# A banded attention and two mixture-of-experts layers on one core: lane weights in halves, other stretches of products, lists inside the third tile, another order of the first units

## The reference

```python
k_sum = k.reshape(B, H, nb, 32, D).max(axis=3); v_sum = v.reshape(B, H, nb, 32, D).mean(axis=3)
# scores: q k^T inside a band of |i-j| < 16, and q k_sum^T + log 32 for the 24 blocks; softmax over both
x = a @ concat(v, v_sum)                      # -> 3072 tokens x 512
# layer 1, closed experts of 384 places: all 3072*8 logits x @ w_gate in falling order,
#   each token goes to the first expert that still has a place
out[mask_e] = relu(x[mask_e] @ w1[e]) @ w2[e]                    # w1 512x1024, w2 1024x512
# layer 2: tokens with x @ w_skip > 0 only, e = argmax(x @ w_gate), gate = softmax at e
out[mask_e] = x[mask_e] + gate * (relu(x[mask_e] @ w1[e]) @ w2[e])
```

## Time and profile before

| | |
|---|---|
| runs without profile | median 840.15 us of 3 (838.03 to 840.93) |
| profiled execution | 839.7 us, its span 837.9 us |
| PE busy | 800.1 us, 95% of the span |
| DVE, ACT, POOL busy | 460.3, 228.3, 214.9 us |
| chain that ended last | PE 76%, DVE 12%, DMA 5%, issue 2%, POOL 2% |
| largest PE groups | L1482 184.0 us, L1496 179.8 us, L1612 102.6 us, L1630 98.8 us |

### The profile page before, as it was taken

The page is one execution under the profiler, slowest core; times in us unless marked ns, Lnnn a source line. Parts: engine busy times, 40 slices in busy tenths (PEclk is TensorE's granted clock), DMA queues, the critical chain, the costliest instruction groups (busy, mean ns, idle before and its releaser), DMA issues.

```text
span 837.9 us, 15121 instructions
## 1 busy us (share of the span) xinstructions
PE 800.1 (95%) x4996; PEld 512.7 (61%) x4996; DVE 460.3 (55%) x2113; ACT 228.3 (27%) x681; POOL 214.9 (26%) x313
## 2 busy tenths in 40 slices
PE   7999998998999999999999999999999999999996
PEld 6778786885445455454554545555576686777762
DVE  7889896777777766667766677516058000000000
ACT  6878786501112021121212212121111111110101
POOL 6888973001030210202102030120300321211110
PEclk9999999999999999999999999999999999999999
DMA  9986650716070622507135070437978999898983
GB/s 252 283 246 206 218 157 6 258 62 222 0 289 26 218 96 71 218 25 264 51 119 194 1 289 25 165 150 278 345 306 330 398 360 348 309 341 305 331 321 115
DMA packets 64505, 171.66 MB, mean 205 GB/s; under 512 B 5584, under 2 KB 5584, under 8 KB 64448
## 3 DMA queue, kind: packets, MB, share of 16 engines
q1 hardware_dynamic: 54512, 143.70, 49.5%
q0 software_dynamic: 6480, 20.91, 6.4%
q10 hardware_dynamic: 3456, 6.29, 2.0%
HBM read 148.41 MB, written 22.81 MB: 204 GB/s over the span
## 4 chain that ended last, share of the span: by engine, by line
PE 76%; DVE 12%; DMA 5%; issue 2%; POOL 2%; SPq 1%; ACT 1%; DVEq 0%; POOLq 0%; ACTq 0%
PE bank L1496 19%; PE bank L1482 16%; PE bank L1630 12%; PE bank L1612 11%; DVE junk L1035 6%; PE bank L1345 3%; PE bank L1372 3%; PE bank L1354 2%; DMA kc<-in_kT 2%; PE bank L1562 1%; DMA weights<-in_moe_w 1%; PE bank L1688 1%; DVE reached L1050 1%; DVE cand L1052 1%; PE bank L1342 1%
## 5 line engine op out<-in xcount | busy, mean ns | idle before, releaser
L1482 PE MATMUL bank<-features,weights 128*128 128x384 f32 x512 | 184.0, 502 | 0.7 <-ACT features L755 0.7
L1496 PE MATMUL bank<-weights 128*128 128x512 f32 x384 | 179.8, 605 | 0.0
L1035 DVE TENSOR_SCALAR_CACHE_REDUCE junk<-Vt,cand 128x192 bf16<-128x192 f32 x376 | 136.2, 410 | 4.8
L1482 PEld LDWEIGHTS bank<-features,weights 128*128 128x128 f32 x512 | 89.1, 191 | 51.2 <-issue 10.4
L1612 PEld LDWEIGHTS bank<-x2T,weights 128*128 128x128 f32 x896 | 102.2, 192 | 5.9 <-issue 5.9
L1612 PE MATMUL bank<-x2T,weights 128*128 128x128 f32 x896 | 102.6, 275 | 0.0
L1496 PEld LDWEIGHTS bank<-weights 128*128 128x128 f32 x384 | 67.1, 190 | 56.8 <-issue 54.5
L1630 PE MATMUL bank<-weights,h2T 128*128 128x512 f32 x224 | 98.8, 593 | 0.4 <-ACT h2T L822 0.4
L1191 DVE SCALAR_TENSOR_TENSOR o<-bank,gate,x 128x512 f32<-128x512 f32 x14 | 10.5, 751 | 155.7 <-PE bank L1630 155.7
L760 ACT ACTIVATE weights<-bank 128x384 f32<-128x384 f32 x64 | 31.4, 490 | 141.2 <-PE bank L1482 141.2
L1630 PEld LDWEIGHTS bank<-weights,h2T 128*128 128x128 f32 x224 | 41.3, 190 | 46.5 <-issue 46.5
(11 more groups left out here) (329 smaller groups left out, 1042.8 us busy)
## 6 DMA issues: line engine op xcount, KB each, us to landing
weights<-in_moe_w SPq DMA_DIRECT2D x52, 2048.0 KB, 10.1
vw<-in_vwin SPq DMA_DIRECT2D x16, 576.0 KB, 4.8
qc<-in_qT SPq DMA_DIRECT2D x16, 384.0 KB, 5.3
kc<-in_kT SPq DMA_DIRECT2D x16, 384.0 KB, 5.9
vc<-in_vT SPq DMA_DIRECT2D x16, 384.0 KB, 7.7
x_rows<-xr SPq DMA_DIRECT2D x24, 256.0 KB, 2.3
y_rows<-weights ACTq DMA_DIRECT2D x24, 256.0 KB, 2.6
weights<-x_rows,gidx POOLq DMA_INDIRECT x24, 6.2
```

The costliest lines, as they stand in the source:

```text
L1035: ins = ve.tensor_scalar(junk[:, c, :], Vt[:, :], cand[:, c:c + 1].bitcast(fp32), 0.0, ALU.is_ge, ALU.add, accum_out=cnt[:, c:c + 1])
L1482: ins = mm(HB[r % 2][:, 0:CAP], w1[:, c, 128 * r:128 * r + 128], xgT[:, c, :], start=(c == 0), stop=(c == KC - 1))
L1496: ins = mm(YB[j % 2][:, :], hT[:, r, 128 * j:128 * j + 128], w2[:, r, :], start=(r == 0), stop=(r == FC - 1))
```

## The change

It has four parts. (1) In the attention's start PE runs 13 small matmuls on zeros instead of 11 and `scores(1)` stands ahead of `mean_rows(0)`; on DVE `maxima(1)` stands ahead of `block_maxima(1)`. (2) `room(w)` releases other amounts per stretch in windows 2 to 7. (3) `lists2(2, ...)` stands inside the second product of the third tile, ahead of its sixth matmul, and on DVE `token_lists` ahead of `combine2` of the third tile. (4) The lane weights come in two transfers of 1 MB each for w1 and w2, with a semaphore for each half; the shared tile starts on the first half of w1 and waits for the rest ahead of the third of four row blocks, and likewise for w2 ahead of the fifth of eight.

```diff
-                sp.dma_start(weights[:, bass.ds(lane, 1), 0:KC * F].rearrange("p o (c f) -> p (o c) f", c=KC),
-                             w1b[bass.ds(e, 1), :, :].rearrange("o (c p) f -> p (o c) f", p=128)).then_inc(s["w1_lanes"], 16)
+                for h, name in enumerate(("w1_lanes", "w1_rest")):
+                    rows = DM // 2
+                    sp.dma_start(weights[:, bass.ds(lane, 1), KC * F // 2 * h:KC * F // 2 * (h + 1)]
+                                 .rearrange("p o (c f) -> p (o c) f", c=KC // 2),
+                                 w1b[bass.ds(e, 1), rows * h:rows * h + rows, :].rearrange("o (c p) f -> p (o c) f", p=128)) \
+                        .then_inc(s[name], 16)
...
             maxima(0)
+            maxima(1)
             block_maxima(1)
-            maxima(1)
             first_windows(1, 1)
...
             one_hots(NT, NSLOT)
-            combine2(2, 0, 2, 1)
             dve.wait_ge(s["id2_mm"], 2)
             token_lists(ID2P, KA, NSLOT)
+            combine2(2, 0, 2, 1)
...
-            for _ in range(11):
+            for _ in range(13):
                 mm(LG[0:32, 0:128], wg2[:, 0, :], wg2[:, :, :].rearrange("p c e -> p (c e)"), start=True, stop=True)
...
+            scores(1)
             mean_rows(0)
-            scores(1)
             scores(2)
...
-                return [8] + [9, 8] * 7 + [9] * 3 + [15, 28, 4, 8]
+                return [8] + [8] * 6 + [9] * 11 + [14, 28, 4, 8]
...
+                    if f == 5 and third:
+                        lists2(2, NT, NSLOT, ID2P)
...
                 pe.wait_ge(s["w1_lanes"], 16 * LANES)
-                for k in range(KC):
-                    product1(0, k)
+                product1(0, 0)
+                product1(0, 1)
+                pe.wait_ge(s["w1_rest"], 16 * LANES)
+                product1(0, 2)
+                product1(0, 3)
...
                 columns(1)
-                for f in range(2, FC):
+                product2(2)
+                product2(3)
+                pe.wait_ge(s["w2_rest"], 16 * LANES)
+                for f in range(4, FC):
                     product2(f)
```

More of the change, by code:

```diff
@@ L261, in banded_attention_two_moe_layers @@
             onehot_ready blk_ready id_mm idp_ready ids_ready tok_c
-            xg_in0 xg_in1 xg_in2 xg_tr xgT_ready w_in0 w_in1 w_in2 w_in3 w2_in0 w2_in1 w2_in2 w2_in3 w1_lanes w2_lanes h_mm h_act y_mm y_evac y_tr yT_ready l2_mm l2T_ready l2_tr l2_evac y_out y_st y_written
+            xg_in0 xg_in1 xg_in2 xg_tr xgT_ready w_in0 w_in1 w_in2 w_in3 w2_in0 w2_in1 w2_in2 w2_in3 w1_lanes w1_rest w2_lanes w2_rest h_mm h_act y_mm y_evac y_tr yT_ready l2_mm l2T_ready l2_tr l2_evac y_out y_st y_written
             gate_sub gate_exp rows8_ready base8_mm teA_ready onehot2_ready id2_mm gid2_ready route2_ready
@@ L449, in _ @@
                 wait(sp, "h2_mm", 2 * (used + k + 1))
-                sp.dma_start(weights[:, bass.ds(lane, 1), 0:KC * F].rearrange("p o (c f) -> p (o c) f", c=KC),
-                             w1b[bass.ds(e, 1), :, :].rearrange("o (c p) f -> p (o c) f", p=128)).then_inc(s["w1_lanes"], 16)
-                wait(sp, "y2_mm", START + used + k + 1)
-                sp.dma_start(weights[:, bass.ds(lane, 1), KC * F:KC * F + FC * DM].rearrange("p o (c f) -> p (o c) f", c=FC),
-                             w2b[bass.ds(e, 1), :, :].rearrange("o (c p) f -> p (o c) f", p=128)).then_inc(s["w2_lanes"], 16)
+                for h, name in enumerate(("w1_lanes", "w1_rest")):
[4 more added lines that the diff above has]
+                        .then_inc(s[name], 16)
+                wait(sp, "y2_mm", START + used + k + 1)
+                for h, name in enumerate(("w2_lanes", "w2_rest")):
+                    rows, at = F // 2, KC * F + FC * DM // 2 * h
+                    sp.dma_start(weights[:, bass.ds(lane, 1), at:at + FC * DM // 2].rearrange("p o (c f) -> p (o c) f", c=FC // 2),
+                                 w2b[bass.ds(e, 1), rows * h:rows * h + rows, :].rearrange("o (c p) f -> p (o c) f", p=128)) \
+                        .then_inc(s[name], 16)
         @block.gpsimd
@@ L1460, in room @@
                 if w == 2:
-                    return [8] + [9, 8] * 7 + [8] * 3 + [13, 22, 4, 4]
-                return [8] + [9, 8] * 7 + [9] * 3 + [15, 28, 4, 8]
+                    return [8] + [8] * 5 + [9] * 12 + [13, 22, 4, 4]
+                return [8] + [8] * 6 + [9] * 11 + [14, 28, 4, 8]
             def load_x(k, j):
@@ L1614, in layer1, with layer2 @@
                 ins.then_inc(s["h2_mm"], 1)
-            def layer2(b, par, buf, landed, next_buf, next_uses, first=False, shared=False):
+            def layer2(b, par, buf, landed, next_buf, next_uses, first=False, third=False, shared=False):
                 x2_transpose(b + 1, next_buf, next_uses, XB2)
@@ L1720, in _ @@
             for b in range(KA):
-                if b == 3:
-                    lists2(2, NT, NSLOT, ID2P)
                 if b >= 1:
@@ L1725, in _ @@
                     layer1(b, b % 2, b, BEFORE[b] + 1, 1)
-                layer2(b, b % 2, b, BEFORE[b] + 1, (b + 1) % NX, (b + 1) // NX + 1, first=b == 0, shared=b == KA - 1)
+                layer2(b, b % 2, b, BEFORE[b] + 1, (b + 1) % NX, (b + 1) // NX + 1, first=b == 0, third=b == 2, shared=b == KA - 1)
             def tile2(i, c):
```

## The result

| | before | changed |
|---|---|---|
| runs without profile, this comparison | median 840.54 us of 4 (838.03 to 843.49) | median 830.28 us of 4 (829.02 to 831.22) |
| profiled execution, its span | 839.7 us, 837.9 us | 829.02 us, 827.3 us |
| PE busy | 800.1 us, 95% | 796.5 us, 96% |

The ratio is 0.988 with a 95% interval of 0.9856 to 0.9904. In a second comparison the changed kernel had a ratio of 0.9891 (0.9855 to 0.9927), 831.78 against 840.22 us. The forecast was 832.0 us.

The account below looks back on a forecast made before the run. PE, busy for 95% of the span, was taken as the bound, so its idle times count. 0 - 4.1 - 1.9 - 2.0 = -8.0 us from 839.7 gave 831.7, carried to 832.0 us for the median; range 829.9 to 835.0.

Parts of the forecast that it names:

- Part 1, forecast 0: Attention's start: two added matmuls hidden, PE's 1.05 us wait filled, but the fourth unit's keys decide; 0, bounds -0.8 to +0.1.
- the change does not relieve them: Start: transfer engines stay fully taken, so VectorE arrives 0.8 us earlier and waits 1.8 us for the fourth unit's keys.
- Rival (d): Start: the gain counts in full, as PE and not the load sets the pace; -0.8, 831.2 us, chance 0.08.
- the picture of the clock: Start: clock granted at 0.50 behind PE's 1.05 us wait for value sums; after the change it stays at 1.00.
- Part 2, forecast -4.1: First layer's windows: fewer thin rounds; -3.95 in five windows, +0.70 in window 2, -0.86 behind window 7; bounds -2.0 and -4.9.
- the term 5 x 0.79 = 3.95: Windows 3 to 7: thin-round losses fall from 1.71 to 0.92 us, so each of five windows is 0.79 us shorter.
- Rival (c): Windows: they give only the idle the row shows, 0.4 to 0.5 us each; +2, 834 us, chance 0.10.
- Rival (e): Six windows: transposes, 0.86 us nearer the gather, wait for it; at 2 us each 843.7 us, slower, chance 0.02.
- Part 3, forecast -1.9: Second layer: lists inside the third tile send the gather earlier, so PE's whole wait at the fifth tile goes; bounds 0 and -1.9.
- Rival (b): Fifth tile: the wait for its rows stays or moves; up to +1.9, 833.9 us, chance 0.08.
- Part 4, forecast -2.0: Shared tile: with lane weights in halves, PE's waits of 1.03 and 0.74 us go; bounds 0 and -2.1.
- Rival (a): Shared tile: the halves of the lane weights land together; +2.0, 834.0 us, chance 0.10.

Follow-up runs that it names:

- part 1 alone: The kernel before with only the new order of the first units in the attention's start: 838.39 us, ratio 0.9964.
- The refilled rooms: The changed kernel with another table of rooms, meant to leave no round of a window below 1.76 us of TensorE work: 826.43 us, ratio 0.983.
- part 2 alone: The kernel before with only the new amounts of products released per stretch of rounds in the first layer's windows: 834.73 us, ratio 0.9938.
- the run with half of the edit: The kernel before with the list products inside the third tile, but VectorE's combination of that tile still ahead of the token lists: 840.81 us.
- part 4 alone: The kernel before with only the lane weights loaded in halves and the products waiting for each half: 837.91 us, ratio 0.997.
- the four single parts: Four kernels, each the kernel before with one of the change's four parts, in order: 838.39, 834.73, 839.40 and 837.91 us.
- the changed kernel with the old units: The changed kernel with the first units of the start back in the old order, the other three parts kept: 831.00 us, ratio 0.9872.

## Why the prediction was right, and where not

**Part 1, forecast 0.** The total came out near it, but the price of part 1 is not settled, and its reasoning holds in part. That a load decides where the start ends holds in ten of fourteen profiles, in which VectorE waits for the fourth unit's keys; in the other four it is late by itself. The mean time at which it reads them is 26.35 us in five profiles with the new units and unchanged loads (24.59, 28.34, 26.97, 25.20, 26.65) and 26.39 us in six with the old (25.96, 26.06, 26.23, 25.80, 26.97, 27.33). The 1.37 us of the first pair of profiles lies well inside this spread, so they need no cause in the edit. The step "the change does not relieve them" is not contradicted, but samples that spread by 3.75 us could hide a gain of 1 us. The timings point in different directions, 2.4 us faster for part 1 alone and 0.8 slower inside the changed kernel, and leave it open too. Rival (d), a start that counts in full at -0.8, is neither shown nor refuted.

What failed is the picture of the clock. The wait of 1.05 us for the value sums belongs to one profile: in the other five with the old first units it is 0.45 to 0.76 us, and the clock behind it stays at 1.00. With the new units this wait is gone, but the next one, for the windows of the second unit's keys, is 1.4 to 3.2 us. The clock stayed at 1.00 through the start in two of the five profiles with the new units and unchanged loads, and fell to 0.50 for some microseconds in three, two of them behind that wait. So the 1.00 that the prediction gave as a sign came true in the first profile by luck.

**Part 2, forecast -4.1, measured -4.62.** The dealing of items was right: two thin rounds left in a window, the new wait at the threshold (3.18 us), window 2 longer by 0.75 (forecast 0.70), one product less at the end. Mis-sized is the term 5 x 0.79 = 3.95: windows 3 to 6 got shorter by 0.80, 0.94, 0.94 and 0.92 us, and with the last window and the rest behind it (-1.77, forecast -0.79 - 0.86) that is 0.56 more than forecast; where a window's other 0.15 us come from, no run shows. The sum for window 2 counts as a loss of 0.36 a thin round that the text calls kept. Rival (c) is refuted by the stretches: the idle time shown in a window fell from 0.94 to 0.43 us, 0.51 less, and the window got 0.95 shorter. The refilled rooms say the same: a wait is worth nearly twice what the row shows, as the prediction had it from the modelled ends of the matmuls. I then used the shown figures for my own expectation of these rooms, and erred as rival (c) does. Rival (e), a wait for the gather, did not come in the changed kernel; with part 2 alone PE waited once, 0.36 us at 496.53, in window 7. So the slack was smaller than the prediction made it.

**Part 3, forecast -1.9, measured -1.88** in the change and alone. The lists started 6.69 us earlier than 648.70, to a hundredth where the prediction put them on the old scale, and the one-hots end at 641.75, 0.26 us ahead of them. The gather went out 3.93 us later. Rival (b), a wait that stays, is refuted: PE did not wait for the fifth tile's rows. That VectorE's order had to change with it, which the prediction said in one sentence, is shown by the run with half of the edit.

**Part 4, forecast -2.0, measured -2.10** (-2.05 alone). Rival (a) is refuted: in the run with part 4 alone the halves landed 2.6 and 3.5 us apart, in order and in time. The first half of w1 came at 813.8, forecast near 813. The margin of its second half was 0.5 us. The Trainium skill's fixed cost of 2.0 us ("DMA: Bandwidth & Descriptors", Anatomy of one DMA), which the page fits to transfers that GpSimd issues and which the prediction held against SyncE's, did not show between queued transfers: the second halves ended 0.4 and 0.1 us later, counted from the first issue, than the undivided loads, and that of w2 was 2.1 us early.

**What chance gave.** The 2.07 us beyond the sum: 1.37 us in the start, and 0.70 us between the first and the second window. The latter is no part of the change either: this distance is 45.21 us in the profile of before, and 44.5 to 44.6 in those of the four single parts, three of which have the old first units, and 45.24 again in the run with half of part 3. In the profile of before the slowest of 24 stores of token rows landed after 4.4 us (3.6 in the changed kernel), and PE waited for the rows behind it:

```profile
167.82 0.44 PE L1402 MATMUL bank<-ident,xT 128*128 128x128 f32 x2 [0.72 <-ACT xr L750]
```

In the seven profiles where the slowest store took 3.5 to 3.8 us PE did not wait there; in the seven with 3.9 to 4.4 us it waited 0.2 to 0.7 us, old and new units among both. The sum was made against a profile with a slow store. The second pair of the changed kernel gives 840.22 - 831.78 = 8.4 us, close to the 8.0 of the sum.

## What to carry to other kernels

Price a wait from start to start and not by the idle time in the row: here one of 0.2 us cost nearly 0.4. Where work items fill the rounds of another engine's loop, deal them so that no round falls below that loop's time; with the number of items unchanged this gave 4.6 us, and 5.4 more once no round with three tries was thin. When an instruction is moved into a tile, look on every engine at what is queued behind the end of that tile. Before a difference at the start is put down to an edit, take several profiles of the start.

## What the runs showed of the hardware

The second unit's keys, 384 KB, issued at 2.66 us as the fifth transfer of the queue in each of the twelve profiles with that order, were read by VectorE between 9.85 and 11.90 us, in nine of them after a wait for the load. In the two profiles of the changed kernel the whole difference stays to the end. What sets it is open.

A wait of the same length at the same place changes the clock in some executions and not in others. PE waits 1.56 us for GpSimd once between 91.6 and 95.8 us in all fourteen profiles, and in three of them the clock fell behind it. In the changed kernel with the old units it fell (timeline, then the stretch), and in the second profile of the changed kernel it did not:

```profile
94.45 1.04 PE L1361 MATMUL bank<-ident,pr 128*120 128x128 f32 x4 [1.56 <-POOL pr L510]
...
94.00:96.00 2.00, 1.55 (x7) 1.48 (x8) 0.75 (x3) 1.98 (x10) 2.00 (x4) 0.64 1.00 367
```

```profile
93.97 0.65 PE L1361 MATMUL bank<-ident,pr 128*120 128x128 f32 x4 [1.56 <-POOL pr L510]
...
94.00:96.00 2.00, 2.00 (x21) 1.87 (x23) 1.33 (x3) 1.72 (x9) 2.00 (x3) 1.00 1.05 405
```

Four transposes took 1.04 us instead of 0.65, and from them to the first window it was 56.09 us instead of 54.94, 1.15 longer. The Trainium skill says in "TensorE: Matmul & The Clock Gate", What's actually happening, that the monitor runs free of the kernel and the cold stretch of one kernel varies from run to run. It says so of a kernel's start; these rows show the same for a wait in its middle.
